# Raw outputs of the tails in two column halves, step 0's second tile split before its last addition, and up's two banks alternating, in a linear attention followed by two Strassen-Winograd layers

## The reference

```python
kv  = einsum('bhsd,bhse->bhde', k, v)        # 4 batches, 8 heads, 576 tokens, head width 64
out = einsum('bhsd,bhde->bhse', q, kv)
out = out / sqrt(mean(out**2, -1) + 1e-6) * g_norm
x   = out as (2304 tokens, 512)
h = x @ w_in1;  g = h * sigmoid(1.702 * h);  x = g @ w_out1      # d_ff 2048
h = x @ w_in2;  g = softplus(h);             out = g @ w_out2
```

## Time and profile before

| | us |
|---|---|
| median of 3 runs | 817.93 (817.62 to 819.13) |
| the profiled execution | 818.39 |
| its span, first to last instruction | 816.6 |
| PE busy | 805.2 (99%) |
| DVE, ACT, POOL busy | 588.9, 425.0, 223.0 |

### The profile page before, as it was taken

The page is one execution under the profiler, slowest core; times in us unless marked ns, Lnnn a source line. Parts: engine busy times, 40 slices in busy tenths (PEclk is TensorE's granted clock), DMA queues, the critical chain, the costliest instruction groups (busy, mean ns, idle before and its releaser), DMA issues.

```text
span 816.6 us, 12377 instructions
## 1 busy us (share of the span) xinstructions
PE 805.2 (99%) x4604; PEld 734.2 (90%) x4604; DVE 588.9 (72%) x1029; ACT 425.0 (52%) x809; POOL 223.0 (27%) x263
## 2 busy tenths in 40 slices
PE   8989999999999999999999999999999999999998
PEld 7978999999999999999998888898888988989886
DVE  3779767687665786665678777888767889766774
ACT  3773332334221233223246776788767678766765
POOL 4888987304421403254501401100000000000000
PEclk9999999999999999999999999999999999999999
DMA  9936547426455462756642525224433322452402
GB/s 358 405 158 236 213 143 280 159 116 217 159 219 203 154 238 91 246 200 250 231 171 101 206 102 205 107 90 150 164 126 119 152 91 101 159 180 90 149 33 77
DMA packets 24426, 139.78 MB, mean 171 GB/s; under 512 B 2224, under 2 KB 6960, under 8 KB 17200
## 3 DMA queue, kind: packets, MB, share of 16 engines
q1 hardware_dynamic: 24224, 138.95, 46.6%
q10 hardware_dynamic: 144, 0.07, 0.0%
HBM read 104.92 MB, written 34.08 MB: 170 GB/s over the span
## 4 chain that ended last, share of the span: by engine, by line
PE 92%; DVE 3%; ACT 2%; issue 1%; DMA 1%; SPq 0%; ACTq 0%; DVEq 0%
PE ps L640 42%; PE ps L705 23%; PE ps L713 16%; PE ps L710 8%; PE ps L583 1%; DMA kv_in_sb<-k_v 1%; PE ps L566 1%; DVE xs_f L984 1%; DVE gs_f L1013 1%; PE ps L602 0%; DVE ex L1066 0%; DVE rms L953 0%; PE ps L588 0%; DVE gs_f L1069 0%; ACT fix L819 0%
## 5 line engine op out<-in xcount | busy, mean ns | idle before, releaser
L640 PE MATMUL ps<-xs,w_in 128*128 128x384 f32 x2016 | 409.5, 338 | 2.3 <-DVE gs_f L1013 2.0
L640 PEld LDWEIGHTS ps<-xs,w_in 128*128 128x128 f32 x2016 | 356.4, 188 | 27.7 <-issue 4.0
L705 PE MATMUL ps<-w_out,gs 128*128 128x512 f32 x864 | 226.0, 393 | 0.0
L1013 DVE TENSOR_TENSOR gs_f<-ps,gs_f 128x384 f32<-128x384 f32 x240 | 133.2, 555 | 113.7 <-PE ps L640 112.2
L705 PEld LDWEIGHTS ps<-w_out,gs 128*128 128x128 f32 x864 | 160.0, 188 | 23.9 <-issue 0.5
L713 PE MATMUL ps<-gs,w_out 128*128 128x512 f32 x576 | 148.2, 392 | 0.0
L713 PEld LDWEIGHTS ps<-gs,w_out 128*128 128x128 f32 x576 | 105.6, 188 | 16.4
L809 ACT ACTIVATE lg<-gs_f 128x384 f32<-128x384 f32 x73 | 38.3, 526 | 123.2 <-DVE gs_f L1013 122.1
L487 POOL TENSOR_TENSOR w_in<-w_in_f,w_in 128x256 fp32r<-128x256 f32 x112 | 94.1, 876 | 29.1 <-ACT w_in L849 28.9
L844 ACT CAST gs<-gs_f 128x384 fp32r<-128x384 f32 x96 | 48.9, 509 | 67.7 <-DVE gs_f L1073 66.4
L710 PE MATMUL ps<-gs,w_out 128*128 128x256 f32 x576 | 83.9, 281 | 0.1
(11 more groups left out here) (64 smaller groups left out, 576.8 us busy)
## 6 DMA issues: line engine op xcount, KB each, us to landing
w_in<-w_kept SPq DMA_DIRECT2D x40, 1792.0 KB, 7.3
w_kept<-w_in SPq DMA_DIRECT2D x16, 1792.0 KB, 10.8
w_in_f<-w_in SPq DMA_DIRECT2D x16, 512.0 KB, 4.1
w_out_f<-w_out SPq DMA_DIRECT2D x16, 512.0 KB, 9.0
kv_in_sb<-k_v SPq DMA_DIRECT2D x8, 640.0 KB, 10.2
kv_in_sb<-k_v SPq DMA_DIRECT2D x8, 576.0 KB, 11.9
q_sb<-q_t SPq DMA_DIRECT2D x16, 288.0 KB, 10.2
out<-xy SPq DMA_DIRECT2D x18, 256.0 KB, 7.8
```

Source lines behind the costliest of these rows:

```text
L640: mm = nc.tensor.matmul(ps[:, bank, 0:HALF], w[:, wp, W_OF[k], cols], xs[:, k, xp, t], start=(new and t == 0 and (wp, xp) == (HI, HI)), st ...
L705: mm = nc.tensor.matmul(ps[:, acc_bank(1, j), 0:DM], g[:, j * P:(j + 1) * P], w, start=new, stop=done)
L1013: nc.vector.tensor_tensor(to, bank, other, ALU.add).then_inc(added, 1)
```

## The change

- The tails' q is no longer padded: each tail (64 columns of queries) makes 64 rows of its own, the even unit's rows 0 to 63 and the odd one's 64 to 127. The two zero fills on DVE and the waits on them go.
- The raw weights of steps 0 and 1 are loaded one unit later (`W_AT`).
- POOL splits B21 before it makes the sums of weights 1. It makes x's T3 itself (`first_t3`), behind B22, and splits T1 ahead of T3, T2, T4. DVE makes T1 behind unit 8, T2 behind unit 10 (it waits for POOL's T3) and T4 behind unit 11.
- POOL makes the sums of weights 2 behind the wait for g_split, no longer ahead of it.
- Up's banks A and B change places in odd steps; P1 waits for the C21 addition of the step before, P6 for the C12 addition.
- P1 of step 1 runs ahead of P3 of step 0. In step 0 DVE splits tile C11, gates and splits C21, and then makes the C12 addition; ACT takes the sigmoid of C21 ahead of unit 15's gain.

```diff
-            q_sb = sb("q_sb", [P, Q_SLOTS, S + PAD], F32, att)
+            q_sb = sb("q_sb", [P, Q_SLOTS, S], F32, att)
...
-            place = {P2: P6, P6: P2}.get(k, k) if m == 0 else k
+            place = {P2: P6, P6: P2, P3: PRODUCTS}.get(k, k) if m == 0 else -1 if (m, k) == (1, P1) else k
...
-        X_EARLY = (B11, B21, B22, T3, T2, T4, T1)
+        X_EARLY = (B11, B21, B22, T1, T3, T2, T4)
+        X_EARLY_SUMS = (T1, T2, T4)
...
-                if u == 0:
-                    sp.wait_ge(pads_made, 2)
-                first = PAD if u % 2 else 0
-                sp.dma_start(q_sb[:, b, first:first + S], q_t[u]).then_inc(q_in[b], 16)
+                sp.dma_start(q_sb[:, b], q_t[u]).then_inc(q_in[b], 16)
...
-                        sp.wait_ge(prod_done, PRODUCTS * (last + 1))
+                        sp.wait_ge(prod_done, step_done(last))
...
-            W_AT = {0: 0, 5: 1, 11: 2}
+            W_AT = {1: 0, 6: 1, 11: 2}
...
+            def first_t3():
+                a, b, op = x_sum_of(0, T3)
+                nc.gpsimd.tensor_tensor(x_sum(0, T3), a, b, op).then_inc(t3_early, 1)
...
             x_early(B11)
+            x_early(B21)
             w_sums(1)
-            x_early(B21)
             w_high(1)
             w_low(1)
-            for slot in X_EARLY[2:]:
+            x_early(B22)
+            first_t3()
+            for slot in X_EARLY[3:]:
                 x_early(slot)
             w_out_low(0, 0)
+            pool.wait_ge(g_split, C21 + 1)
             w_sums(2)
-            pool.wait_ge(g_split, C21 + 1)
             w_high(2)
...
-                        mm = nc.tensor.matmul(out_rows[:, FULL_ROWS:FULL_ROWS + P], tail,
-                                              kv_sb[:, v % UNIT_SLOTS, :], start=(v != u), stop=(v == u))
+                        rows = slice(TAIL, P) if v == u else slice(0, TAIL)
+                        mm = nc.tensor.matmul(out_rows[rows, FULL_ROWS:FULL_ROWS + P], tail,
+                                              kv_sb[:, v % UNIT_SLOTS, :], start=True, stop=True)
...
-                bank = BANK_B if k in (P6, P7, P4) else BANK_A
+                bank = bank_b(m) if k in (P6, P7, P4) else bank_a(m)
...
-                        pe.wait_ge(added, ADDS * (m - 1) + C12_ADD + 1)
+                        pe.wait_ge(added, ADDS * (m - 1) + C21_ADD + 1)
+                if k == P6 and m > 0:
+                    pe.wait_ge(added, ADDS * (m - 1) + C12_ADD + 1)
...
             turn(UNITS - 1)
+            product(1, P1)
             product(0, P3)
...
+                if u == UNITS + 1:
+                    hidden(0, C21)
...
-                if u == 2 * PAIRS + 1:
-                    dve.wait_ge(x_made, 2 * PAIRS)
-                    raw_x(0, T3)
+                if u == 2 * PAIRS:
+                    dve.wait_ge(x_made, PAIRS + 2)
+                    raw_x(0, T1)
+                if u == 2 * PAIRS + 2:
                     raw_x(0, T2)
-                if u == 2 * PAIRS + 2:
+                if u == 2 * PAIRS + 3:
                     raw_x(0, T4)
-                if u == 2 * PAIRS + 3:
-                    raw_x(0, T1)
...
                 if m == 0:
                     gate_split(m, C11)
-                    add(m, C12_ADD)
...
-                    gate_product(m, C21)
-                    if m > 0:
-                        gate_split(m, C21)
-                if m > 0:
-                    add(m, C12_ADD)
+                    gate(m, C21)
+                add(m, C12_ADD)
...
-                if m == 0:
-                    gate_split(m, C21)
```

More of the change, by code:

```diff
@@ L68, in build @@
     FULL_ROWS = MAIN * P
-    PAD = P - TAIL
     HALF = 384
@@ L129, in build @@
         cleared = sem("cleared")
-        pads_made = sem("pads_made")
         kv_done = sem("kv_done")
@@ L153, in build @@
         x_raw_made = sem("x_raw_made")
+        t3_early = sem("t3_early")
         x_hi_made = sem("x_hi_made")
@@ L206, in q_tokens @@
         def q_tokens(u, slot):
-            main = slice(P, P + FULL_ROWS) if u % 2 else slice(0, FULL_ROWS)
-            tail = slice(0, P) if u % 2 else slice(FULL_ROWS, FULL_ROWS + P)
+            main = slice(TAIL, S) if u % 2 else slice(0, FULL_ROWS)
+            tail = slice(0, TAIL) if u % 2 else slice(FULL_ROWS, S)
             return q_sb[:, slot, main], q_sb[:, slot, tail]
@@ L234, in build, with bank_a, bank_b, step_done @@
         P1_UNIT, P2_UNIT = 10, 12
+        def bank_a(m):
+            return BANK_B if m % 2 else BANK_A
+        def bank_b(m):
+            return BANK_A if m % 2 else BANK_B
         def products_done(m, k):
-            place = {P2: P6, P6: P2}.get(k, k) if m == 0 else k
+            place = {P2: P6, P6: P2, P3: PRODUCTS}.get(k, k) if m == 0 else -1 if (m, k) == (1, P1) else k
             return PRODUCTS * m + place + 1
+        def step_done(m):
+            return max(products_done(m, k) for k in range(PRODUCTS))
         def split_buffer(d):
@@ L302, in x_raws @@
         def x_raws(ci, slot):
-            return 4 * ci + X_RAW_ORDER.index(slot) + 1
+            if ci == 0:
+                return X_EARLY_SUMS.index(slot) + 1
+            return len(X_EARLY_SUMS) + 4 * (ci - 1) + X_RAW_ORDER.index(slot) + 1
         def x_his(ci, slot):
@@ L573, in raw_output @@
                 q_slot = u % Q_SLOTS
-                if u == 0:
-                    pe.wait_ge(pads_made, 2)
                 pe.wait_ge(q_in[q_slot], 16 * (u // Q_SLOTS + 1))
@@ L738, in _ @@
                 for k in range(PRODUCTS):
-                    product(m, k)
+                    if (m, k) != (1, P1):
+                        product(m, k)
                     down(m - 1, came, shares(m)[k])
@@ L787, in first_product @@
                     wait_down(act, m - 2)
-                nc.scalar.copy(hid(m, C21), ps[:, BANK_A, 0:HALF]).then_inc(t1_made, 1)
+                nc.scalar.copy(hid(m, C21), ps[:, bank_a(m), 0:HALF]).then_inc(t1_made, 1)
             def keep_c11():
@@ L801, in hidden @@
                     act.wait_ge(prod_done, products_done(m, P2))
-                    h = ps[:, BANK_A, 0:HALF]
+                    h = ps[:, bank_a(m), 0:HALF]
                 else:
@@ L916, in _ @@
                     round_x(ci + 1, T3)
-                hidden(m, C21)
+                if m > 0:
+                    hidden(m, C21)
                 if ends:
@@ L942, in _ @@
         def _(dve):
-            nc.vector.memset(q_sb[:, 0:Q_SLOTS:2, S:S + PAD], 0.0).then_inc(pads_made, 1)
-            nc.vector.memset(q_sb[:, 1:Q_SLOTS:2, 0:PAD], 0.0).then_inc(pads_made, 1)
             nc.vector.memset(eps_col[:], EPS).then_inc(cleared, 1)
@@ L978, in raw_x @@
                     dve.wait_ge(x_split, x_splits(ci - 1, T1))
-                if slot == T2:
+                if slot == T2 and ci == 0:
+                    dve.wait_ge(t3_early, 1)
+                elif slot == T2:
                     dve.wait_ge(x_raw_made, x_raws(ci, T3))
@@ L991, in add @@
             def add(m, which):
-                a, b = ps[:, BANK_A, 0:HALF], ps[:, BANK_B, 0:HALF]
+                a, b = ps[:, bank_a(m), 0:HALF], ps[:, bank_b(m), 0:HALF]
                 p1 = hid(m, C21)
@@ L1039, in hidden_of @@
             def hidden_of(m, tile):
-                return ps[:, BANK_A, 0:HALF] if tile == C11 and m > 0 else hid(m, tile)
+                return ps[:, bank_a(m), 0:HALF] if tile == C11 and m > 0 else hid(m, tile)
             def gate(m, tile):
```

## The result

The changed kernel takes 821.23 us (median of 7 runs, 819.47 to 822.03), the kernel before 817.73 (7 runs, 817.58 to 819.13). The ratio is 1.0034 [1.0023, 1.0045], so it is 0.34% slower. Forecast were 820.1 us, in a range of 816.8 to 821.4. The profiled execution is one of the fastest of the seven, 819.62 us with a span of 817.8, against 818.39 and 816.6 before.

A forecast was written before the change was run, and what follows sets the result against it. PE bounds the kernel, with nearly all its idle time ahead of down(0). The terms -0.5 - 1.0 + 2.64 + 1.2 - 0.2 = +2.1 us against the 817.93 median give 820.1 us; range 816.8 to 821.4.

The forecast's parts named there:

- The stall: At down(1), PE waits 2.64 us for POOL's w_out 1, delayed by sums 2 behind g_split; ends 2.0 and 3.0.
- Rival 2: From g_split to w_out 1, POOL runs faster without DVE contention and is in time: -1.7, 816.2 us; chance 0.12.
- The clock: Behind PE's idle stretch at down(1), the granted clock falls to half: +1.2 us, ends 0 and 1.6.
- rival 1: At down(1), PE stalls but the clock doesn't fall: +0.9, 818.9 us; chance 0.33.
- a sign of being wrong: Anywhere in the kernel, PE idle in a place that the prediction doesn't name; no size given.
- Up to down(0): Start to down(0): 0.5 us won earlier plus 1.0 at step 0's end, putting down(0) at 61.9 instead of 63.38.
- I take 0.5 us won up to here: DVE, units 10 to 12: T2 0.8 us earlier than T4 before, 0.3 given back; ends 1.4 won, 1.2 lost.
- Rival 3: In the attention, POOL's T3 is 1.7 us later than taken: 821.8 us with the clock, 820.6 without; chance 0.10.
- The start: Units 2 to 8: later weights loads; landings limit PE's lead to 0.7 us at unit 3, 0.55 at unit 8.
- Tails: Odd attention units: half-array tail products take 0.25 us instead of 0.45, 0.2 less per pair while PE sets the pace.
- rival 4: Attention tails don't run side by side, 0.4 us later at x_made: 820.5 us, or 819.3 with clock kept; chance 0.08.
- Banks: Past 63 us, alternating up's banks removes P1's wait for C12, 0.21 us at 458.06: -0.2; ends -0.6 and 0.

The follow-up runs named there:

- second: Kernel before with only the sums of weights 2 moved behind POOL's wait for g_split; 821.51 us, ratio 1.004.
- the third experiment: Kernel before with alternating banks, P1 of step 1 ahead of P3, and C21's sigmoid, gate and split earlier; 817.00 us, ratio 0.9985.
- the first experiment: Changed kernel with the sums of weights 2 put back ahead of POOL's wait for g_split; 818.39 us, ratio 0.9999.
- the sixth experiment: Changed kernel with POOL splitting w_out 1 ahead of sums 3 and making high parts 3 in place of ACT; 821.88 us, ratio 1.0043.
- the ninth: The third experiment with DVE making one x sum behind each of units 8 to 11 (T1, T3, T2, T4); 816.06 us, ratio 0.9978.
- the eighth experiment: Kernel before with only the tails in two halves and weights 0 and 1 loaded one unit later; 818.97 us, ratio 1.0008.
- fourth: The first experiment with T3 made by DVE behind unit 9 instead of by POOL; 817.46 us, ratio 0.9989.

## Why the prediction was right

**The stall** was the main term and is shown. 2.64 us were forecast and 2.53 measured; POOL's unbroken stretch was forecast at 18.5 us and is 18.6. The move alone costs 3.1 us, and taking it back removes the wait. Rival 2, POOL in time, is refuted. Low parts 2 did take less (5.66 against 6.11), but sums 2 took 3.6, not 3.25, and so nothing was shed. That the stall itself agrees to 0.1 us is in part luck: PE's way to down(1), taken as unchanged at 15.8, was 16.1, and this made up for POOL's longer chain.

**The clock** was the largest doubt. The fall is real, but not in every execution: the forecast's mechanism is what the long ones do, and rival 1's (no fall) what the shortest do, at 819.5 to 819.6 where it had 818.9. The row that I took the fall from is itself one of two kinds: at the same place, behind 1.68 and 1.67 us of idle time, the profiles of the second and third experiments show no fall. Against the profiled execution of before I had +0.9 without a fall and +2.1 with one; measured are +1.2 and, with both falls, +3.6. The fall was mis-sized, 1.54 where I took 1.2, though inside my end of 1.6. A second idle stretch of 1.75 us, at unit 13's raw output, has its own fall at times, 0.46 us. I had said that this product waits for DVE behind T2, and priced no fall of the clock there. PE's 0.79 us ahead of P6, for POOL's split, I had not named at all, and by my own list that is a sign of being wrong. The remaining 0.4 us of that execution lie behind down(2), and I have no cause for them. The median, 821.23 at a clock of 0.997, would fit the execution without a fall and the larger fall alone, 819.62 + 1.54 = 821.16. This is not shown, since no execution near the median was profiled, and the two profiled ones without a fall are 0.63 apart. On that reading, that it lies 1.1 over the forecast is 0.3 by the size of the fall and 0.3 by the steps (+1.2 for +0.9); the rest is about the 0.46 by which I had set the profiled execution of before over the median, which did not carry over to the changed kernel. Why is open. Between the medians the change is +3.5 us (821.23 - 817.73) where +2.1 was forecast, and the median lies inside the range by only 0.2 us. By the Trainium skill (TensorE: Matmul & The Clock Gate, "HAM oscillation") neither gap should cost clock. The rows above disagree, with 0.50 granted behind 1.78 and 2.51 us of idle time.

**Up to down(0)** the sum was right (61.9 forecast, 61.81 measured). I gave 0.5 us to what lies ahead of the end of step 0 and 1.0 to the end itself. The C21 addition came at 57.79 in place of 58.06, 0.27 earlier, and from there to C21's split it is 3.93 us in place of 5.22, 1.29 less. The edit's own part of this is the 1.0 that I took (1.05 in the third experiment); the rest is contention, told below. The weak step is "I take 0.5 us won up to here": the 0.27 hang on a unit 8 that started 0.85 early in this execution, the start alone wins no time, and with sums 2 ahead of the wait the full change is 1.4 us behind the third experiment (818.39 against 817.00). T2 ended at 43.76, 0.22 earlier than T4 in its place before, where 0.8 was forecast. It came at 42.21, where 41.4 was forecast. Three things are in that: low parts 1 at 5.58, not 4.86 (an end that I had named, for the earlier trace rows), B21 at 24.77 instead of 24.5, and T3 itself as priced (1.81 for 1.83). Rival 3's mechanism is there in part: T3 is 0.7 us late, not the 1.7 that it asked for.

**Contention** is the term that was missing. I costed sums 2 only where they went, not what they did where they stood. In the kernel before they stretched C11's gate product to 0.79 us (at 58.54), and with them gone it took 0.55: this 0.24 hid in the agreement at 61.8. With POOL and DVE as the changed kernel has them, they would cost the gates 0.96 ahead of the wait, and that made me expect too much of the first experiment.

**The start**: the bound by landings, 0.55 us at unit 8, was passed in this execution (0.85), by no more than the landings scatter. That nothing of it comes through was right: the start and the tails alone win no time.

**Tails**: I took 0.2 us in each pair. Here is one odd unit before and one in the changed kernel: the raw output's eight products, the tails, and the next unit's k and v.

```profile
22.46 1.15 PE L583 MATMUL ps<-kv_sb,q_sb 128*128 128x128 f32 x8
23.45 0.61 PE L588 MATMUL ps<-kv_sb,q_sb 128*128 128x128 f32 x4
...
24.54 0.80 PE L566 MATMUL ps<-kv_in_sb 128*64 128x64 f32 x20
```

```profile
21.50 1.16 PE L600 MATMUL ps<-kv_sb,q_sb 128*128 128x128 f32 x8
22.59 0.44 PE L607 MATMUL ps<-kv_sb,q_sb 128*64 128x128 f32 x4
...
23.65 0.80 PE L585 MATMUL ps<-kv_in_sb 128*64 128x64 f32 x20
```

The tail group is shorter, 0.44 for 0.61 (0.37 for 0.45 from its start to the next group's). But it starts 1.09 us behind the raw output, not 0.99, and the transposes behind it take 0.70 for 0.64. So from raw output to k and v the unit takes 2.15 us in place of 2.08. The halves win nothing even where PE sets the pace, which is rival 4's case. Its price of 0.4 us doesn't show at down(0).

**Banks**: the wait at 458 us is gone. A like one that I had overlooked, 0.20 us at 447.34 in the kernel before, stays, with 0.18 at 448.69. From down(1) to the end of the span the changed kernel takes 737.3 us and the one before 737.4, where I took 0.2 less.

## What to carry to other kernels

Before a piece of a helper engine's work is moved behind a wait, add its length to that engine's unbroken chain up to its next due time: here 3.25 us went into 0.61 of slack, and having POOL idle beside the gates was worth 1 us at most. In the sixth experiment, which gave the helper another order and 1.9 us more work, the wait came out one step later. What helped in the ninth was to spread DVE's sums evenly over the units, so that PE's next product was never behind two of them. When two profiles are compared, set them level at a point ahead of all edits first: 0.6 of the 1.63 us in the third experiment lay there. Where an edit brings TensorE a new idle stretch like the ones here, count half clock behind it in some of the executions.

## What the runs showed of the hardware

- Behind the same idle time the granted clock falls to 0.50 in some executions and stays at 1.00 in others: 1.67 to 1.69 us at 10.5 us (one fall in three profiles of kernels alike up to there), 1.75 to 1.79 at 46 and 2.51 to 2.53 at 80.5 to 81 (both in two of four profiles of the changed kernel). It cost 0.46 us at 46 us and 1.54 at 81.
- Elementwise work of GpSimd and VectorE on SBUF slows both. A 128x384 low part took 0.56 us on DVE alone and 0.98 beside POOL's sums. POOL's seven 128x256 low parts of weights 1 took 4.86 us in the kernel before, the third and the eighth experiment, and 5.57 to 5.59 in the changed kernel and the first, fourth and ninth, where DVE's T1 runs beside them.
- Two products of 64 columns of weights, on two halves of the array and with 64 output rows each, took 0.37 us from the group's start to the next group's, where the two full ones took 0.45, and the groups around them took 0.16 more.
- The landing of a load under a full queue scatters: unit 8's k and v were used between 26.21 and 26.95 us in kernels that are the same up to there.
